# Attention scores contracted over one head's 64 rows at a time instead of over 128 rows with zero-padded keys

## The reference

```python
block, window = (32, 16)
k_sum = k.reshape(B, H, nb, block, D).max(axis=3)       # 24 block keys per head
v_sum = v.reshape(B, H, nb, block, D).mean(axis=3)
scores_l = scale * np.matmul(q, k.transpose(0, 1, 3, 2))
mask_l = np.abs(pos[:, None] - pos[None, :]) < window
scores_s = scale * np.einsum('bhsd,bhnd->bhsn', q, k_sum) + np.log(block)
scores_all = np.concatenate([np.where(mask_l, scores_l, -1e9), scores_s], axis=-1)
a = softmax(scores_all)
out = np.matmul(a, np.concatenate([v, v_sum], axis=2))
```

## Time and profile before

| | |
|---|---|
| three runs | 696.98, 699.44 and 1279.12 us; median 699.44 us |
| span of the profiled execution | 693.3 us, from first to last instruction |
| TensorE busy in the span | 660.6 us (95%) |
| weight loads busy | 551.9 us (80%) |
| VectorE, ScalarE, GpSimd busy | 285.0, 219.7, 68.9 us |
| TensorE's mean granted clock | 0.963 of full |
| attention stage | from the start to about 167 us |

### The profile page before, as it was taken

One profiled execution on the slowest core, in us unless ns is written; L12 is line 12 of the kernel. 1 busy time (PEld: TensorE's weight loads), 2 busy tenths in 40 slices (PEclk: granted clock), 3 DMA queues, 4 the chain that ended last, 5 costly groups with the idle time before them and its releaser, 6 DMA issues.

```text
span 693.3 us, 11440 instructions
## 1 busy us (share of the span) xinstructions
PE 660.6 (95%) x3329; PEld 551.9 (80%) x3330; DVE 285.0 (41%) x780; ACT 219.7 (32%) x504; POOL 68.9 (10%) x81
## 2 busy tenths in 40 slices
PE   5999999999889599999999999999999999999993
PEld 3888888889868488888888788888888888888882
DVE  2665555544487312542214565532432222322221
ACT  2554545442245321442214443321211111111111
POOL 2200000001235300020000010000300002000002
PEclk9999999998569799999999999999999999999997
DMA  7532333101476911541011553320100001000001
GB/s 174 116 86 71 89 90 87 45 17 61 168 274 184 187 55 45 170 148 45 30 45 47 171 162 107 91 77 6 70 17 1 0 1 44 17 0 0 0 0 61
DMA packets 73100, 53.01 MB, mean 76 GB/s; under 512 B 46816, under 2 KB 59376, under 8 KB 73072
## 3 DMA queue, kind: packets, MB, share of 16 engines
q1 hardware_dynamic: 65760, 36.38, 20.0%
q10 hardware_dynamic: 4320, 7.87, 3.5%
q0 software_dynamic: 2992, 8.42, 3.2%
HBM read 40.57 MB, written 12.07 MB: 76 GB/s over the span
## 4 chain that ended last, share of the span: by engine, by line
PE 90%; DMA 3%; DVE 3%; issue 1%; POOL 1%; ACT 0%; ACTq 0%; DVEq 0%; SPq 0%
PE ps L760 9%; PE ps L762 9%; PE ps L761 9%; PE ps L569 5%; PE ps L541 5%; PE ps L778 5%; PE ps L776 5%; PE ps L777 5%; PE ps L568 4%; PE ps L696 3%; PE ps L698 3%; PE ps L697 3%; PE ps L669 3%; PE ps L671 3%; PE ps L670 3%; PE ps L526 2%
## 5 line engine op out<-in xcount | busy, mean ns | idle before, releaser
L760 PE MATMUL ps<-x2T,wm 128*128 (+1 forms) x288 | 112.1, 389 | 0.5 <-issue 0.5
L762 PE MATMUL ps<-x2T,wm 128*128 (+1 forms) x288 | 112.1, 389 | 0.0
L761 PE MATMUL ps<-x2T,wm 128*128 (+1 forms) x288 | 112.0, 389 | 0.0
L1424 DVE TENSOR_TENSOR sg<-sg,ps 128x512 f32<-128x512 f32 x36 | 24.7, 687 | 99.4 <-ACT sg L1008 96.5
L760 PEld LDWEIGHTS ps<-x2T,wm 128*128 128x128 f32 x288 | 54.1, 188 | 12.0 <-issue 0.9
L762 PEld LDWEIGHTS ps<-x2T,wm 128*128 128x128 f32 x288 | 54.1, 188 | 11.3
L761 PEld LDWEIGHTS ps<-x2T,wm 128*128 128x128 f32 x288 | 54.1, 188 | 11.2
L776 PE MATMUL ps<-wm,h2T 128*128 128x512 f32 x144 | 56.8, 394 | 0.0
L778 PE MATMUL ps<-wm,h2T 128*128 128x512 f32 x144 | 56.2, 390 | 0.0
L777 PE MATMUL ps<-wm,h2T 128*128 128x512 f32 x144 | 56.1, 389 | 0.0
L1008 ACT ACTIVATE sg<-ps 128x512 f32<-128x512 f32 x36 | 21.5, 598 | 100.0 <-PE ps L762 100.0
(11 more groups left out here) (182 smaller groups left out, 1080.3 us busy)
## 6 DMA issues: line engine op xcount, KB each, us to landing
raw<-in_moe_w_dram SPq DMA_DIRECT2D x24, 512.0 KB, 5.6
xin<-x_in_slots ACTq DMA_DIRECT2D x16, 256.0 KB, 2.7
y_sorted<-ysb ACTq DMA_DIRECT2D x14, 256.0 KB, 2.1
qn<-in_q_dram SPq DMA_DIRECT2D x16, 192.0 KB, 2.9
kn<-in_k_dram SPq DMA_DIRECT2D x16, 192.0 KB, 3.1
v<-in_v_dram SPq DMA_DIRECT2D x48, 64.0 KB, 2.0
raw<-in_moe_w_gate_dram SPq DMA_DIRECT2D x12, 256.0 KB, 3.0
raw<-in_moe_w_val_dram SPq DMA_DIRECT2D x12, 256.0 KB, 3.2
```

The lines of the kernel that those rows point to most:

```text
L760: mm(o, hi, xh, start=(kk == 0), stop=False)
L761: mm(o, hi, xl, start=False, stop=False)
L762: last = mm(o, lo, xh, start=False, stop=(kk == KD - 1))
```

## The change

- kT loses its two padded planes: it is one plane of 128 rows, head 0 above head 1, and the zeros, their memsets on GpSimd and TensorE's wait for them go.
- Each step has four scores matmuls instead of two: for head 0 the 160 local keys, then the 24 block keys, with rows 0 to 63 of qT and kT; then the same for head 1 with rows 64 to 127. Head 0 writes PSUM bank 2 and head 1 bank 3, in each step.
- So a step's scores wait for the masking of the step before (`masked`, 2 * count) instead of the one before that; VectorE waits for both heads' scores before it masks.
- ScalarE copies k in two pieces instead of four (at t = 2 and t = 4). VectorE writes block maxima straight into kT; ksum and its copies (L1064) go.
- The counts of the semaphores follow, and the transposes of the gate that use bank 2 wait for the masking of all 48 steps instead of 47.

```diff
-                    wait(pe, masked, 2 * (count - 1))
-                    lhsT = qT[:, s, t * P:(t + 1) * P]
-                    o = ps[:, 2 + n % 2, 0:2 * COLS].rearrange("p (h c) -> p h c", h=2)
-                    mm(o[:, :, 0:KEYS], lhsT, kT[:, s, :, KEY0[t]:KEY0[t] + KEYS], start=True, stop=True)
-                    if t == 0:
-                        pe.wait_ge(k_ready, 2 * (unit + 1))
-                    mm(o[:, :, KEYS:COLS], lhsT, kT[:, s, :, S:KTW], start=True, stop=True).then_inc(scores_done, 1)
+                    for hh in range(2):
+                        if hh == 0:
+                            wait(pe, masked, 2 * count)
+                        rows = slice(hh * D, (hh + 1) * D)
+                        lhsT = qT[rows, s, t * P:(t + 1) * P]
+                        mm(ps[:, 2 + hh, 0:KEYS], lhsT, kT[rows, s, KEY0[t]:KEY0[t] + KEYS], start=True, stop=True)
+                        if t == 0 and hh == 0:
+                            pe.wait_ge(blocks_maxed, 2 * (unit + 1))
+                        mm(ps[:, 2 + hh, KEYS:COLS], lhsT, kT[rows, s, S:KTW], start=True, stop=True).then_inc(scores_done, 1)
...
             def copy_k(unit, s, piece):
-                hh, bank = piece % 2, piece // 2
-                rows, cols = slice(hh * D, (hh + 1) * D), slice(bank * 512, min(bank * 512 + 512, S))
+                cols = slice(piece * 512, min(piece * 512 + 512, S))
                 act.wait_ge(k_turned, unit + 1)
-                if piece == 2:
+                if piece == 1:
                     act.wait_ge(blocks_maxed, 2 * unit + 1)
-                nc.scalar.copy(kT[rows, s, hh, cols], turned[rows, cols]).then_inc(k_copied, 1)
+                nc.scalar.copy(kT[:, s, cols], turned[:, cols]).then_inc(k_copied, 1)
...
-                    for piece in {2: (0,), 3: (1,), 4: (2, 3)}.get(t, ()):
+                    for piece in {2: (0,), 4: (1,)}.get(t, ()):
                         copy_k(unit + 1, (n // TQ + 1) % 2, piece)
...
-                V.tensor_reduce(ksum[:, lo // BLOCK:hi // BLOCK],
+                V.tensor_reduce(kT[:, s, S + lo // BLOCK:S + hi // BLOCK],
                                 turned[:, lo:hi].rearrange("q (n w) -> q n w", w=BLOCK),
                                 AX, ALU.max).then_inc(blocks_maxed, 1)
...
-                    dve.wait_ge(scores_done, count + 1)
-                    wait(dve, probs_ready, 2 * (count - 2))
+                    dve.wait_ge(scores_done, 2 * (count + 1))
+                    if not before:
+                        wait(dve, probs_ready, 2 * (count - 2))
...
-                        V.tensor_tensor_reduce(sm[:, n % 3, hh, :], ps[:, 2 + n % 2, hh * COLS:(hh + 1) * COLS],
+                        V.tensor_tensor_reduce(sm[:, n % 3, hh, :], ps[:, 2 + hh, 0:COLS],
```

More of the change, by code:

```diff
@@ L191, in build @@
         kn, at = place("kn", at, [P, TQ, 2, D], F32)
-        ksum, at = place("ksum", at, [P, NB], F32)
-        kT, at = place("kT", at, [P, 2, 2, KTW], F32)
+        kT, at = place("kT", at, [P, 2, KTW], F32)
         qT, at = place("qT", at, [P, 2, S], F32)
@@ L240, in build @@
         q_turned, k_turned = sem("q_turned"), sem("k_turned")
-        q_copied, k_copied, blocks_maxed, k_ready = sem("q_copied"), sem("k_copied"), sem("blocks_maxed"), sem("k_ready")
+        q_copied, k_copied, blocks_maxed = sem("q_copied"), sem("k_copied"), sem("blocks_maxed")
         means_done, means_copied, means_spread = sem("means_done"), sem("means_copied"), sem("means_spread")
@@ L407, in _ @@
         def _(pool):
-            for hh in range(2):
-                nc.gpsimd.memset(kT[(1 - hh) * D:(2 - hh) * D, :, hh, :], 0.0).then_inc(zero_filled, 1)
-                pool.wait_ge(zero_filled, hh + 1)
             nc.gpsimd.memset(zeros[:], 0.0).then_inc(zero_filled, 1)
@@ L420, in spread_means @@
                 nc.gpsimd.tensor_copy(v2_unit, vsum[rows].unsqueeze(1).broadcast_to([NB, TQ, 2 * D])).then_inc(means_spread, 1)
-            pool.wait_ge(zero_filled, 3)
+            pool.wait_ge(zero_filled, 1)
             spread_means(0)
@@ L501, in turn_q @@
                 pe.wait_ge(q_in, 32 * (unit + 1))
-                wait(pe, k_copied, 4 * unit)
+                wait(pe, k_copied, 2 * unit)
                 wait(pe, blocks_maxed, 2 * unit)
@@ L534, in step @@
                         pe.wait_ge(q_copied, 2 * (unit + 1))
-                        pe.wait_ge(k_copied, 4 * unit + 2)
+                        pe.wait_ge(k_copied, 2 * unit + 1)
                     elif t == 1:
-                        pe.wait_ge(k_copied, 4 * (unit + 1))
-                    wait(pe, masked, 2 * (count - 1))
-                    lhsT = qT[:, s, t * P:(t + 1) * P]
-                    o = ps[:, 2 + n % 2, 0:2 * COLS].rearrange("p (h c) -> p h c", h=2)
-                    mm(o[:, :, 0:KEYS], lhsT, kT[:, s, :, KEY0[t]:KEY0[t] + KEYS], start=True, stop=True)
-                    if t == 0:
-                        pe.wait_ge(k_ready, 2 * (unit + 1))
-                    mm(o[:, :, KEYS:COLS], lhsT, kT[:, s, :, S:KTW], start=True, stop=True).then_inc(scores_done, 1)
+                        pe.wait_ge(k_copied, 2 * (unit + 1))
+                    for hh in range(2):
[7 more added lines that the diff above has]
+                        mm(ps[:, 2 + hh, KEYS:COLS], lhsT, kT[rows, s, S:KTW], start=True, stop=True).then_inc(scores_done, 1)
                 if n >= 2 and not (static and n - 2 >= NSTEP):
@@ L582, in _ @@
             turn_k(0)
-            pe.wait_ge(zero_filled, 2)
             for n in range(0, 6):
@@ L592, in gate_turn @@
                 if j == GT:
-                    pe.wait_ge(masked, 2 * (NSTEP - 1))
+                    pe.wait_ge(masked, 2 * NSTEP)
                 elif j > 0:
@@ L829, in step @@
                 if not (static and n // TQ >= NSTEP // TQ - 1):
-                    for piece in {2: (0,), 3: (1,), 4: (2, 3)}.get(t, ()):
+                    for piece in {2: (0,), 4: (1,)}.get(t, ()):
                         copy_k(unit + 1, (n // TQ + 1) % 2, piece)
-            for piece in range(4):
+            for piece in range(2):
                 copy_k(0, 0, piece)
@@ L1045, in copy_q, with max_blocks @@
                 V.tensor_copy(qT[:, s, cols], turned[:, cols]).then_inc(q_copied, 1)
-            def max_blocks(unit, bank):
+            def max_blocks(unit, s, bank):
                 dve.wait_ge(k_turned, unit + 1)
[L1051 to L1054, removed]
+                if bank == 0:
+                    dve.wait_ge(k_copied, 2 * unit + 1)
                 lo, hi = bank * 512, min(bank * 512 + 512, S)
-                V.tensor_reduce(ksum[:, lo // BLOCK:hi // BLOCK],
+                V.tensor_reduce(kT[:, s, S + lo // BLOCK:S + hi // BLOCK],
                                 turned[:, lo:hi].rearrange("q (n w) -> q n w", w=BLOCK),
                                 AX, ALU.max).then_inc(blocks_maxed, 1)
[L1060 to L1064, removed]
             def copy_means(unit):
@@ L1129, in step @@
                     elif t < 5 and t > 2:
-                        max_blocks(unit + 1, 4 - t)
-                    if t == 4:
-                        copy_ksum(unit + 1, 1 - (n // TQ) % 2)
+                        max_blocks(unit + 1, 1 - (n // TQ) % 2, 4 - t)
             copy_q(0, 0, 0)
             copy_q(0, 0, 1)
-            max_blocks(0, 1)
-            max_blocks(0, 0)
-            copy_ksum(0, 0)
+            max_blocks(0, 0, 1)
+            max_blocks(0, 0, 0)
             for n in range(0, 6):
```

## The result

The changed kernel took 717.33 us (median of 4 runs, 710.98 to 721.69) against 698.21 us: ratio 1.028, 95% interval 1.024 to 1.032. Its profiled execution has a span of 716.3 us, 23.0 more than before, and a mean granted clock of 0.927 in place of 0.963. The time is 2.0 us above the forecast of 715.3 and inside the range. The reasons behind the forecast were wrong all the same: at the full clock the change makes the attention stage *faster*. The medians hold all executions, but the ratios leave out those over 1.5% above the fastest of the same kernel: one of the four here, 16 of the 58 of the kernel before beside the experiments (706 to 714 us, mean clock 0.941 to 0.950, none traced), and up to half of a variant's.

The account below looks back on a forecast made before the run. TensorE, never idle in the attention stage, was taken as the bound. Step costs of 3.76 + 8.50 + 1.29 + 2.30 gave +15.8 us: span 693.3 to 709.1, plus 6.1 around it 715.3 us; range 708 to 726.

Parts of the forecast that it names:

- rival 1: Attention scores: the two heads' loads and streams run side by side, 480 ns less a step, 692.7 us; chance 0.06.
- a wait on the masking: Scores waiting for the previous step's masking: slack 0.65 us, no cost; if gone, each late 0.1 costs 4.7 us; chance 0.03.
- What bounds the kernel: Attention stage: TensorE has no idle time, so its added work is paid in full and savings on other engines are unseen.
- The prices: TensorE at full clock: 0.83 ns a streamed column, 107 a load, 96 for a change in the number of rows.
- an entry in the same mode: Scores after L569: 56 and 64 rows count as one mode, so the entry goes from 256 ns to 107, -149.
- The step that failed: Scores body: eight loads and streams in program order, one load ahead, 969 + x ns against 641 + x; chance 0.52.
- the +328: Scores in every step: ns added from first score stream to first L552 stream, before the differing entries.
- rival 4: Clock: more loads and empty time make it fall by step 45, +12.8 us, 728 us, more in main stage; chance 0.10.
- the start: First block-key matmul: its chain loses about 1.0 us, TensorE's scores left grow by the same; step 0 nets nothing.

## Why the prediction was right in its number and wrong in its reasons

**The number was luck in part.** The forecast was +15.8 us of span; measured were +23.0, by other causes. It then added 6.1 us for what lies around the span, but 693.3 and 699.44 are of different executions: in every execution on record with both figures, the time is 1.6 to 1.7 us above the span. With 1.7 the sum gives 710.8 us for the profiled execution, and it took 718.0. Two smaller slips changed nothing: rival 1 takes 480 off a step, so its 336 is a share of 480 and not of 393; and the 0.03 for a wait on the masking, 4.7 us, belonged above the border.

**What bounds the kernel** was right: TensorE is never idle from step 6 to step 46, and all it waited for on other engines in the stage was the q copy, 1.2 us, as before 1.1.

**The prices** held. L569 to the next load is 0.36 between different row counts; L567 to L539 in the changed kernel is 0.28 (63.61 to 63.89), as counted for an entry in the same mode, so going from 56 to 64 rows costs no empty array. The eight padded matmuls cost 0.23 a step, 0.21 by the prices, and grouping the v matmuls gave 0.23 to 0.26, 0.30 by the prices.

**The step that failed** is the sentence "If loads and streams go in program order with one load ahead, as all rows here do". The rows of before could only show matmuls that share rows. With disjoint rows the body is 0.60 us from record to record, and putting both heads in the same rows gave the serial one back. In place of the +328 the scores came out some 200 ns shorter, 0.60 instead of 0.80 us. A step after the v matmuls went from 2.61 to 2.36 or 2.37, -0.25, where the forecast said +0.18 and rival 1 said -0.30. Over a unit the forecast was +1.9 us, rival 1 -0.95, measured -0.77. Rival 1, held at 0.06, was the mechanism, and its argument against, the program order, was void: TensorE took head 1's local keys ahead of head 0's block keys. The rule cited there from the Trainium skill (TensorEngine Tiling (Array Packing), Key Properties) agrees with the trace after, where the first streams of the two heads start 6 ns apart.

**The clock**, rival 4 at 0.10, happened at the same time and was worth about +27 us. "Against: streams of a step are the same" was the flaw: the columns are the same in sum, but once the heads run side by side the local keys pass in 0.32 us in place of the 0.54 of the earlier trace rows. Rivals 1 and 4 were priced each alone; the second follows from the first. 15.8 us of serial work that didn't come were replaced by -6 and +27. Of the latter, what brings the fall in the main stage (9.4 us) is shown by the runs with half and with double columns. The later start of the full clock (23.9 us instead of 13.8) and the gate part (13.3 us) are the clock too, but their cause isn't settled, nor that it is the change: kernels with a full clock in the main stage and with padded 128-row matmuls lost them just as well, one program falls in either group, and neither more streaming nor splitting the logits moved it. Whether the kernel before loses as much in some of its own executions is open as well, as none of over 706 us was traced.

**The other terms** held: the masking wait never showed, the start brought no gain, and the rest of the kernel was 1.9 us longer, not examined.

## What to carry to other kernels

Matmuls on disjoint halves of the rows did run beside each other in these traces, even past ones that stand between them, and a change between 128 rows and 56 or 64 costs about 0.1 us of empty array and opens a load: group them by rows before you count on either. Work that is saved on a busy TensorE can come back as a lower clock, so look at the granted clock by stage before and after; here removing half the score columns alone made the stage slower, and the change brought its 6 us in the main stage only once some 0.25 us of other time had gone from each step in both kernels. In the whole kernel even that is 1%, less than can be told from no change. And when two rivals have a common cause, price them together.

## What the runs showed of the hardware that was not expected

- Loads in different halves of the rows run beside each other: 0.055 us apart in the changed kernel and 7 ns apart with the heads interleaved, where loads in the same rows, 128 or 56 of them, come every 0.107.
- With all scores in rows 0 to 63 TensorE was busy all the time from step 6 to step 47 and stayed at 1.2 GHz until 350 us; with the same columns in eight matmuls over 128 rows it was at 2.4 GHz from 24.7 us on, in the kernel before from 13.8 on.
- The mean granted clock over steps 6 to 41 was 1.00 with the score streams of the kernel before, over 128 rows, and with doubled ones in two halves at a time; 0.91, 0.89 and 0.98 with half of that, in a step after the v matmuls of 2.31 to 2.37 us; and 1.00 again with half of it in such a step of 2.03 to 2.08 us.
- In the gate part the same program lost the full clock 13.6 or 27.2 us after step 42 in two traced executions (688.6 and 684.1 us); its other executions lie at 681 to 684 and 689 to 693 us, but for one of 815.
